# Routed experts on one TensorE: the transposes of h's second half and of the next tile's rows are moved behind the second product of the down-projection

## The reference

```python
# 1: linear attention with a random-feature map, 8 heads of 64
q_p, k_p = (phi(q), phi(k))
num = einsum('bhsf,bhfd->bhsd', q_p, einsum('bhsf,bhsd->bhfd', k_p, v))
attn = num / den
# 2: a causal convolution of 5 taps as a gate
x = (sigmoid(conv(x)) * (x @ w_val)) @ w_out
# 3: one expert for each token, chosen by argmax of x @ w_gate, or held from the token before
for b, s:
    h = maximum(x[b, s] @ w1[e], 0)          # 512 -> 1024
    out[b, s] = p[e] * (h @ w2[e])           # 1024 -> 512
```

## Time and profile before

| | us |
|---|---|
| median of 3 runs | 594.37 (593.65 to 596.05) |
| the profiled execution: its own time | 596.32 |
| the profiled execution: span from first to last instruction | 594.6 |
| TensorE matmul busy in that span | 554.7 (93%) |
| VectorE / ScalarE / GpSimd busy | 310.2 / 268.5 / 216.9 |
| mean granted TensorE clock | 0.982 |

### The profile page before, as it was taken

The page is one execution under the profiler, slowest core; times in us unless marked ns, Lnnn a source line. Parts: engine busy times, 40 slices in busy tenths (PEclk is TensorE's granted clock), DMA queues, the critical chain, the costliest instruction groups (busy, mean ns, idle before and its releaser), DMA issues.

```text
span 594.6 us, 12965 instructions
## 1 busy us (share of the span) xinstructions
PE 554.7 (93%) x5189; PEld 469.4 (79%) x5189; DVE 310.2 (52%) x491; ACT 268.5 (45%) x463; POOL 216.9 (36%) x218
## 2 busy tenths in 40 slices
PE   4999999999979999999949999999999999999994
PEld 4888878787868999678838888888888888888883
DVE  3276776767686555285424555621456665542121
ACT  2245556564566621363524556522456555532221
POOL 2019898989979930437410100010000011000100
PEclk9999999999989999999979999999999999999998
DMA  8233635535440000008924665531356666411110
GB/s 308 89 119 119 197 98 180 165 106 187 129 153 2 1 1 2 0 1 247 290 101 139 216 239 167 195 106 53 96 187 192 207 210 208 141 39 49 35 52 21
DMA packets 30231, 75.04 MB, mean 126 GB/s; under 512 B 3311, under 2 KB 3439, under 8 KB 30192
## 3 DMA queue, kind: packets, MB, share of 16 engines
q1 hardware_dynamic: 23536, 58.73, 30.9%
q0 software_dynamic: 3200, 9.46, 4.2%
q10 hardware_dynamic: 3456, 6.32, 3.9%
HBM read 57.94 MB, written 17.61 MB: 127 GB/s over the span
## 4 chain that ended last, share of the span: by engine, by line
PE 90%; DVE 2%; ACT 2%; issue 2%; DMA 2%; POOL 0%; ACTq 0%; SPq 0%; POOLq 0%; DVEq 0%
PE turn L507 10%; PE turn L508 10%; PE turn L509 10%; PE num_ps L507 7%; PE num_ps L508 7%; PE num_ps L509 7%; PE pair_ps L516 6%; PE kv_ps L550 6%; PE num_ps L563 6%; PE pair_ps L697 3%; PE pair_ps L507 3%; PE pair_ps L509 3%; PE pair_ps L508 3%; PE turn L492 2%; PE turn L502 2%
## 5 line engine op out<-in xcount | busy, mean ns | idle before, releaser
L469 POOL DMA_INDIRECT out_rows<-o_sb,meta_cur x22 | 25.5, 1159 | 262.9 <-DVE o_sb L1112 262.9
L443 POOL TENSOR_TENSOR gate<-gate,tap 128x576 f32<-128x576 f32 x64 | 93.1, 1454 | 5.3
L1103 DVE TENSOR_TENSOR h_t<-pair_ps,h_t 128x512 fp32r<-128x512 f32 x44 | 30.4, 692 | 115.3 <-ACT h_t L899 115.3
L967 DVE TENSOR_TENSOR wts<-stage,wts 128x1024 fp32r<-128x1024 f32 x64 | 75.7, 1218 | 10.9 <-ACT wts L842 10.9
L507 PE MATMUL num_ps<-wts,y_t 128*128 128x512 f32 x176 | 72.6, 412 | 1.5 <-DVE y_t L1094 1.5
L507 PE MATMUL turn<-wts,h_t 128*128 128x512 f32 x176 | 73.2, 416 | 0.0
L842 ACT CAST wts<-stage 128x1024 fp32r<-128x1024 f32 x64 | 65.1, 1048 | 12.7 <-PE turn L509 11.1
L508 PE MATMUL num_ps<-wts,y_t 128*128 128x512 f32 x176 | 70.5, 401 | 0.0
L509 PE MATMUL num_ps<-wts,y_t 128*128 128x512 f32 x176 | 70.4, 400 | 0.0
L508 PE MATMUL turn<-wts,h_t 128*128 128x512 f32 x176 | 69.7, 396 | 0.0
L509 PE MATMUL turn<-wts,h_t 128*128 128x512 f32 x176 | 69.6, 395 | 0.0
(11 more groups left out here) (158 smaller groups left out, 1045.7 us busy)
## 6 DMA issues: line engine op xcount, KB each, us to landing
stage<-in_w SPq DMA_DIRECT2D x64, 512.0 KB, 4.6
kq_t<-in_kq SPq DMA_DIRECT2D x16, 576.0 KB, 6.0
sorted_rows<-padrow SPq DMA_DIRECT2D x9, 771.0 KB, 5.8
ysl<-sorted_rows ACTq DMA_DIRECT2D x24, 257.0 KB, 2.7
v_sb<-in_v_aug SPq DMA_DIRECT2D x16, 325.0 KB, 3.1
wout_t<-in_w_out_t SPq DMA_DIRECT2D x1, 1024.0 KB, 8.1
wval_sb<-in_w_val SPq DMA_DIRECT2D x1, 1024.0 KB, 10.1
wout_sb<-in_w_out SPq DMA_DIRECT2D x1, 1024.0 KB, 12.3
```

Of the source, the lines that this page charges most:

```text
L443: nc.gpsimd.tensor_tensor(g, g, tap[:, t % 2, :], ALU.add).then_inc(conv_step, 1)
L967: nc.vector.tensor_tensor(lo, whole, hi.bitcast(F32), ALU.subtract).then_inc(signal, 1)
```

## The change

In a tile of the experts, TensorE's order of three pieces is altered. Before, it is `turn_y(t + 1)`, `down(0)`, `turn_h(t, 1)`, `down(1)`. Now it is `down(0)`, `down(1)`, `turn_h(t, 1)`, `turn_y(t + 1)`. The two groups of four transposes that stood apart stand directly behind one another. No instruction is added or removed, and the waits stay with the pieces that they belong to.

```diff
@@ -724,12 +724,12 @@
                 turn_h(t, 0)
                 up(1, 2)
                 up(1, 3)
-                turn_y(t + 1)
                 pe.wait_ge(o_read, t + 1)
                 pe.wait_ge(ht_ok, t * 2 + 1)
                 down(0)
+                down(1)
                 turn_h(t, 1)
-                down(1)
+                turn_y(t + 1)
                 down(2)
                 down(3)
                 pe.wait_ge(ht_ok, t * 2 + 2)
```

## The result

| | before | after |
|---|---|---|
| median, 6 runs each | 594.58 us (593.65 to 596.24) | 600.57 us (598.97 to 602.40) |
| ratio after / before | | 1.0098, 95% interval 1.0078 to 1.0119 |
| the profiled execution: own time, span | 596.32, 594.6 | 600.32, 598.6 |

The changed kernel is 1.0% slower: 6.0 us against a forecast of 7.0. The two spans differ by only 4.0 us, because in this execution the part in front of the experts, which the change doesn't touch, was 2.4 us shorter (the first product of the experts starts at 306.41 instead of 308.80). Two differences in that part are large enough to make it up: the wait for the first input DMA was 4.9 us instead of 6.0, and the granted clock between 173 and 182 us averaged 0.81 instead of 0.62. So whole tiles are compared.

The account below looks back on a forecast made before the run. TensorE, busy in all 12.52 us of each tile, was taken to bound the kernel. A gap of 0.32 us in 22 tiles, other terms nothing, adds 7.0 us to the median 594.37: 601.4 us, range 598.6 to 604.0.

Parts of the forecast that it names:

- The gap of 0.32 in a tile: In front of `down(0)`, whose weight load waits for VectorE's half 0 of `h_t`: a gap of 0.32 us a tile.
- 22 times the same gap: Over all 22 tiles, the gap before `down(0)` was taken as 0.32 us in each, 7.0 us in sum.
- The low end of the range: Cheap bound at `down(0)`, weights loaded ahead of the wait: gap of 0.21 us a tile, 4.6 us, 599.0 us.
- Nothing at `down(4)`: Wait of `down(4)` for half 1 of `h_t`: 0.10 us to spare, costed at nothing.
- The first rival: At `down(4)`, the second wait bites too: 0.02 to 0.10 us a tile, 0.4 to 2.2 us; chance 0.13.
- the term of `down(0)`: Wait of `down(0)` for half 0 of `h_t`, uncovered when `turn_y` leaves: 0.32 us a tile, bounds 0.21 to 0.40.
- Nothing for the group: In the transposes, one group of eight saves 0 against two of four, at most 0.09 us a tile.
- The rival of the change-over: In the transposes, switching from products and back is a group's true cost: 2.6 us faster, 591.8 us; chance 0.05.
- the one of cheaper runs: Transposes in a run cheaper, or `down(0)` weights loaded ahead of the wait: both give 597.0 us; chance 0.09.
- No clock loss: In the experts' tiles the clock stays at 1.00; a fall would cost some 3 us, chance 0.03.
- `y_t`: Next tile's rows, made by VectorE behind half 1 of `h_t`: 1.40 us to spare stays, nothing to pay.
- One sign: In the changed profile, idle time before the first load of `down(0)` is put down to VectorE's L1103, 22 times.

Follow-up runs that it names:

- e1: Against the changed kernel, `turn_h(t, 1)` and `turn_y(t + 1)` put back before `down(1)`, so only `turn_y` has moved: 601.46 us, 1.0130 of before.
- e3: Changed kernel with `down(0)`'s wait split, so only its third matmul waits for VectorE's part of `h_t`: 593.94 us, 1.0004 of before.
- e5: Changed kernel with `turn_h(t, 0)` one matmul earlier, before the last matmul of `up(1, 1)`: 596.71 us, 1.0043 of before.
- e2: Against the changed kernel, `turn_y(t + 1)` put back in front of `down(0)`, so only `turn_h(t, 1)` has moved: 601.14 us, 1.0120 of before.
- e4: Changed kernel with `turn_y(t + 1)` one product later, behind `down(2)`, giving three groups of transposes: 602.45 us, 1.0150 of before.
- e8: Same kernel as e4 (changed kernel, `turn_y(t + 1)` behind `down(2)`), timed again beside the changed kernel: 600.91 us, 1.0116 of before.
- e6: Kernel before with `turn_h(t, 1)` cut in two around one matmul of `down(1)`, giving four groups: 593.43 us, 0.9995 of before.
- e9: Kernel before with only `turn_h(t, 1)` moved behind `down(1)`, and `down(4)`'s wait split so its third matmul waits for VectorE: 593.73 us, 0.9994 of before.

## Why the prediction was right

- **The gap of 0.32 in a tile.** Its three parts came out as put down: half 0 of `h_t` late by 0.34 (532.57 against 532.23), 0.12 for the release (0.11 taken), 0.33 to the second matmul (0.33 taken). The release was put behind the end of the separate wait instruction, and there the load stands (532.6 and 51 ns, then 532.69). Tiles of 12.84 were forecast; they are 12.84 and 12.85. That this is the cause is shown by e1 (the move that uncovers it costs all), e3 (the wait split, the loss gone) and e5 (the gap follows the moment of readiness).
- **The term that was mis-sized: 22 times the same gap.** In the tiles that are an expert's first (seven of the 20) it is 0.27 to 0.28, not 0.32 (12.79 and 12.80 against 12.52). There the load starts 0.07 after VectorE's end and not 0.12, for example in the tile from 334.04:

```profile
339.49 0.69 DVE L1103 TENSOR_TENSOR h_t<-pair_ps,h_t 128x512 fp32r<-128x512 f32 x1 [1.58 <-ACT h_t L899]
...
340.26 0.19 PEld L507 LDWEIGHTS turn<-wts,h_t 128*128 128x128 f32 x1 [0.45 <-issue]
```

  The waits for `w_lo` and `ht_ok` come in one instruction in these tiles, which may be why, but no run tests that. Over 20 tiles it is 6.16 us instead of 6.4; for 22, at the same mean, 6.8. The measured 6.0 with its interval (4.6 to 7.1 us) holds this.
- **Two slips and a misreading in the sum, none of which decides it.** 530.58 less 530.27 is 0.31 and not 0.32, which makes 6.8 us and 601.2; 8 x 0.01 is 0.08 and not 0.09. The low end of the range, 0.21, has no ground in the earlier trace rows: the matmuls around 286.38 start at 286.25, 286.48 and 286.72, their usual 0.23 apart, so nothing waited there, and the 0.34 is where that pace put the second matmul, not the price of a wait. That the gap came out near the middle of the range owes nothing to this bound.
- **Nothing at `down(4)`.** 0.10 to spare was forecast, 0.10 it is, with no idle time. e2 shows what it costs once that cover is gone: with 0.44 less between, 0.26 in a tile. The first rival fell. It was also priced too high: the 0.14 of lateness that stays unseen, which the term of `down(0)` contains, was left out of it. By what e2 and e5 show, an estimate, a load 0.10 late would have cost nothing, and this wait was 0.18 and not 0.04 away from costing anything.
- **Nothing for the group.** Eight transposes cost twice 0.44. e4, e8 and e6 change the number of groups from two to three and from three to four, and the tiles don't grow. The rival of the change-over and the one of cheaper runs fell with it. The 0.10 of the earlier trace rows was no quicker pace either: of the four steps between its five loads the first is 0.06 (185.85 to 185.91) and the others are 0.11. The Trainium skill (TensorE: Matmul & The Clock Gate, Back-to-back issue gap) gives about 81 ns for a matmul of 128 columns in a sustained stream; these float32 transposes don't reach it, their loads keep a pace of 0.11, also eight in a row.
- **No clock loss.** The granted clock is 1.00 in all 20 tiles with a gap in each.
- **`y_t`** was to keep 1.40 to spare. It ends at 537.64 and its load comes at 539.03: 1.39. That tiles with a weight chunk keep nearly as much was argued only from their length; in the trace the least of any whole tile is 1.32.
- **One sign was described wrongly.** I wrote that the idle time would be put down to VectorE's L1103. It is put down to "issue", since the wait is an instruction apart from the load. Only e2's gap carries VectorE's name.

## What to carry to other kernels

Where one engine is busy without a hole, an order can't gain by grouping unless a group has a fixed cost, and it loses wherever a piece leaves that stood between a producer's end and its wait. Before such a move, list for each wait the producer's end, the release and the natural start of the waiting load, and see which piece fills the time. In this kernel a load that came late by 0.46, 0.40 and 0.23 us (changed kernel, e2, e5) cost its lateness less 0.14. A wait that comes too early for a product of split operands can be put in front of the one matmul that reads the late part: here this gives 0.47 us of cover for nothing, and makes orders equal that otherwise differ by 1%. It didn't beat the kernel before, since TensorE is busy in all of a tile there.

## What the runs showed that I had not expected

- Four groups instead of three (e6) and e9's order give tiles of 12.51 instead of 12.52, 0.27 us over 20 tiles. It is far below what a time can tell, and no run here looks for its cause.
- The idle time in PEld's row overstates such a gap and PE's row understates it: 0.50 us of idle load queue and 0.09 of hole in PE's busy time (12.84 less 12.75) for a true 0.32, since a late load still overlaps and a matmul's modelled end reaches past the next start.
- The first tile, which has the lower clock (1.2 GHz) in part of it, was between 14.0 us (e9) and 15.7 us (e1) long from one execution to the next, and the experts began between 305.2 and 308.8 us. That is more than many changes are worth, and speaks for comparing windows of whole tiles.
